# The second head's exponential as two activations, each with its own row sum

## What is computed

```python
B, H, S, D = q.shape          # 4, 8, 1152, 64
q_pool = q.reshape(B, H, S // 2, 2, D).mean(axis=3)
scores = scale * np.matmul(q_pool, k.transpose(0, 1, 3, 2))
scores = scores - np.max(scores, axis=-1, keepdims=True)
attn = np.exp(scores)
attn = attn / (np.sum(attn, axis=-1, keepdims=True) + 1e-09)
out = np.matmul(attn, v)      # then moe(out) and mlp(...)
```

## Time and profile before

| | us |
|---|---|
| median of 3 runs | 886.7 |
| lowest and highest of the 3 | 885.58, 887.46 |
| the profiled execution | 885.63 |
| its span in the trace | 883.8 |
| length of a pair in the middle of attention | 32.9 |

### The profile page before, as it was taken

How to read it: one execution, slowest core, us unless ns; L and a number is a source line. 1 busy time by engine, 2 the same in 40 slices (tenths; PEclk the granted TensorE clock), 3 DMA queues, 4 the chain that set the end, 5 groups by cost and what they waited for, 6 DMA issues and landing times. The chain is left out here.

```text
span 883.8 us, 16411 instructions
## 1 busy us (share of the span) xinstructions
PE 811.5 (92%) x5819; PEld 597.8 (68%) x5819; DVE 531.0 (60%) x984; ACT 483.5 (55%) x729; POOL 248.6 (28%) x154
## 2 busy tenths in 40 slices
PE   3899999999999999999999988878678999999998
PEld 3676776776667677676677665634236888888886
DVE  2666666666666766766766754430037667677663
ACT  2566566566566566566566554220048666766672
POOL 2304304404404403403403300000038344334432
PEclk9999999999999999999999999979889999999999
DMA  5353303303303303303303164348960000000000
GB/s 134 131 145 81 81 2 82 80 1 80 80 0 80 80 0 80 80 0 80 80 0 80 63 252 162 125 170 315 404 253 1 25 24 24 24 24 24 24 24 24
DMA packets 82160, 75.49 MB, mean 85 GB/s; under 512 B 42448, under 2 KB 60880, under 8 KB 81616
## 3 DMA queue, kind: packets, MB, share of 16 engines
q1 hardware_dynamic: 79792, 74.47, 26.5%
q10 hardware_dynamic: 2336, 0.59, 0.3%
HBM read 70.32 MB, written 4.72 MB: 85 GB/s over the span
## 5 line engine op out<-in xcount | busy, mean ns | idle before, releaser
L493 ACT ACTIVATE prob<-ps,neg_max 128x1152 f32<-128x1152 f32 x144 | 175.7, 1221 | 186.6 <-DVE spare L402 186.6
L290 PE MATMUL ps<-ident,prob 128*128 128x128 f32 x1296 | 169.7, 280 | 29.3 <-ACT prob L493 27.1
L290 PEld LDWEIGHTS ps<-ident,prob 128*128 128x128 f32 x1296 | 140.7, 142 | 72.5 <-ACT prob L493 63.9
L306 PE MATMUL ps<-probT,v_nat 128*64 128x256 f32 (+1 forms) x1152 | 153.6, 411 | 0.0
L398 DVE TENSOR_REDUCE part_neg<-ps 128x1 f32<-128x512 f32 x160 | 109.7, 692 | 45.7 <-PE ps L259 38.2
L372 DVE COPY probT<-ps 128x128 f32<-128x128 f32 (+1 forms) x192 | 75.5, 421 | 99.5 <-PE ps L290 99.5
L466 ACT ACTIVATE probT<-ps 128x512 f32<-128x512 f32 x208 | 117.1, 594 | 32.1 <-PE ps L290 32.0
L208 POOL TENSOR_TENSOR kT<-k_raw,ones 128x1152 fp32r<-128x1152 f32 x15 | 31.6, 2107 | 311.0 <-DVE k_raw L448 311.0
L259 PE MATMUL ps<-kT,qT_hi 64*128 64x512 f32 (+1 forms) x768 | 112.2, 369 | 2.6 <-DVE qT_lo L389 2.6
L306 PEld LDWEIGHTS ps<-probT,v_nat 128*64 128x64 f32 x1152 | 77.3, 136 | 52.2 <-issue 5.7
L963 PE MATMUL ps<-w_hi,g_even 128*128 128x512 f32 x320 | 102.6, 392 | 2.2 <-POOL g_even L1047 2.0
(11 more groups left out here) (144 smaller groups left out, 1038.5 us busy)
## 6 DMA issues: line engine op xcount, KB each, us to landing
slot<-in_moe_w SPq DMA_DIRECT2D x16, 2048.0 KB, 12.8
v_nat<-in_v SPq DMA_DIRECT2D x16, 576.0 KB, 5.0
k_nat<-in_k SPq DMA_DIRECT2D x30, 288.0 KB, 4.0
q_nat<-in_q SPq DMA_DIRECT2D x32, 256.0 KB, 4.1
out<-res SPq DMA_DIRECT2D x18, 256.0 KB, 2.0
slot<-in_moe_w_in SPq DMA_DIRECT2D x2, 2048.0 KB, 20.8
slot<-in_moe_w_out SPq DMA_DIRECT2D x8, 512.0 KB, 16.7
q_nat_r<-in_q SPq DMA_DIRECT2D x32, 32.0 KB, 3.5
```

Source lines behind the costliest of these rows:

```text
L290: last = nc.tensor.transpose(dst[:, n * P:(n + 1) * P], prob[h][:, kt * P:(kt + 1) * P], ident[:])
L306: last = nc.tensor.matmul(ps[64 * h:64 * h + D, VBANK, 0:n], v_nat[par][:, h, kt, :], probT[g][:, kt, h, :], start=(kt == 0), stop=(kt == ...
L493: nc.scalar.activation(prob[h][:], row, ACT.Exp, bias=neg_max[:, j:j + 1], scale=-1.0, accum_out=sums).then_inc(exp_done, 1)
```

## The change

In every round with two heads, the second head's exponential becomes two activations: columns 0 to 511 with the sum into `row_sum`, raising a new semaphore `exp_begun`, and columns 512 to 1151 with the sum into a new small tile `rest_sum`, raising `exp_done`. On PE head 1's first four transposes (chunk 0) wait for `exp_begun`, and its fifth (the first of chunk 1) for `exp_done`. Head 0 and the mix round are as they were. The two sums are added in `invert`, where a tensor_scalar becomes a scalar_tensor_tensor. POOL fills the two new tiles at the start with zeros, and the waits on `zeroed` go from 4 to 6. In the changed kernel L290 is L298, L466 is L474, L493 is L502 with the second piece at L505, and L256 and L259 of before are L259 and L262.

```diff
+        rest_sum = [sb(f"rest_sum{i}", [P, QT + 1, 2]) for i in range(2)]
...
             for i in range(2):
                 nc.gpsimd.memset(row_sum[i][:], 1.0).then_inc(zeroed, 1)
+                nc.gpsimd.memset(rest_sum[i][:], 0.0).then_inc(zeroed, 1)
             nc.gpsimd.memset(ones[:], 1.0).then_inc(zeroed, 1)
-            pool.wait_ge(zeroed, 4)
+            pool.wait_ge(zeroed, 6)
...
                 tau = tiles_of(p, r) + h
-                pe.wait_ge(exp_done, tau + 1)
+                if h == 0:
+                    pe.wait_ge(exp_done, tau + 1)
                 for c in (2, 0, 1) if r == MIX else range(NCH):
                     dst = turned(r, h, c)
+                    if h == 1 and c == 0:
+                        pe.wait_ge(exp_begun, doubles_of(p, r) + 1)
+                    elif h == 1 and c == 1:
+                        pe.wait_ge(exp_done, tau + 1)
...
-                nc.vector.tensor_scalar(row_den[:], row_sum[par][:], 1e-9, None, ALU.add).then_inc(den_done, 1)
+                nc.vector.scalar_tensor_tensor(row_den[:], row_sum[par][:], 1e-9, rest_sum[par][:], ALU.add, ALU.add).then_inc(den_done, 1)
...
+                first = BANK if h == 1 else S
                 row = flat[:, 3 * h * BANK:3 * h * BANK + S]
-                nc.scalar.activation(prob[h][:], row, ACT.Exp, bias=neg_max[:, j:j + 1], scale=-1.0, accum_out=sums).then_inc(exp_done, 1)
+                nc.scalar.activation(prob[h][:, 0:first], row[:, 0:first], ACT.Exp, bias=neg_max[:, j:j + 1], scale=-1.0,
+                                     accum_out=sums).then_inc(exp_begun if h == 1 else exp_done, 1)
+                if h == 1:
+                    nc.scalar.activation(prob[h][:, first:S], row[:, first:S], ACT.Exp, bias=neg_max[:, j:j + 1], scale=-1.0,
+                                         accum_out=rest_sum[par][:, ROUND[r], h:h + 1]).then_inc(exp_done, 1)
```

More of the change, by code:

```diff
@@ L100, in attention @@
         scores_full, neg_done, exp_done = sem("scores_full"), sem("neg_done"), sem("exp_done")
+        exp_begun = sem("exp_begun")
         ktr_full, qtr_full, q_evac, q_high, q_low = (
@@ L317, in turn_out @@
                 last.then_inc(otr_full, 1)
-            pe.wait_ge(zeroed, 4)
+            pe.wait_ge(zeroed, 6)
             pe.wait_ge(ident_ready, 1)
@@ L382, in _ @@
         def _(dve):
-            dve.wait_ge(zeroed, 4)
+            dve.wait_ge(zeroed, 6)
             split(dve, 0)
@@ L468, in _ @@
             load_k(act, 0)
-            act.wait_ge(zeroed, 4)
+            act.wait_ge(zeroed, 6)
             nc.scalar.activation(warm[:], ones[:], ACT.Exp)
@@ L1139, in program @@
                ("outT0", 2 * P + QR), ("outT1", 2 * P), ("ones", 8), ("warm", 8), ("part_neg", 8), ("spare0", P), ("neg_max", 16),
-               ("row_sum0", 16), ("row_sum1", 16), ("mix_sum0", 8), ("mix_sum1", 8), ("row_den", 16), ("row_inv", 16)),
+               ("row_sum0", 16), ("row_sum1", 16), ("rest_sum0", 16), ("rest_sum1", 16), ("mix_sum0", 8), ("mix_sum1", 8), ("row_den", 16), ("row_inv", 16)),
     }
```

## The result

The changed kernel takes 875.68 us (median of 4 runs, 874.87 to 877.19) where the kernel before takes 886.14 (4 runs, 884.62 to 887.46) beside it: a ratio of 0.9884, 95% interval 0.9862 to 0.9907. It was run again later: 875.91 us (6 runs), ratio 0.9888, interval 0.9851 to 0.9926. So it is faster by 10 us, 1.2%. The forecast was 879.0 with a range from 876.0 to 883.5: the right direction and, for most of the gain, the right mechanism, but the gain was over a third larger than forecast (10.5 us against 7.7) and the time lies just under the range.

A forecast was written before the change was run, and what follows sets the result against it. PE bounds the kernel, through its work and gaps in attention. 16 pairs at 0.49 us, less 0.18, give 7.7 us; 886.7 - 7.7 = 879.0 us, forecast case 877.9 to 880.8, range 876.0 to 883.5.

The forecast's parts named there:

- The bound and the ceiling: Attention on PE: blocks of 18 loads against 1.94 us unhindered lose 0.67 us a pair, at most 10.7 us over 16 pairs.
- d: ACT, head 1's exponential: the fixed part of an activation's pitch, which the second activation repeats, taken as 0.25 us.
- The blocks: PE's 18 loads in rounds 0, 1, 3, 4: end at old release + 0.25 + 0.53 us or unhindered, whichever is later.
- The tightest place: Round 1, ACT's copy out of bank 0 before the next scores: covered by only 0.02 us, so nothing lost.
- The sum of the blocks: Attention's 16 pairs at 0.49 us each, less 0.18 for the first pair's round 0: 7.7 us faster.
- Does the rest follow: Everything outside the blocks: copies covered, exponentials move along, the part behind attention moves with its end; no further loss.
- a cheaper activation: Rival on ACT: shorter activations overlap more, d near 0.19, gain 9.5 us, 877.2 us, down to 876; chance 0.12.
- a gain given back: Rival: round 1's gain runs into bank 0 and is lost, gain 4.8 us, 881.9 us, up to 883.5; chance 0.13.
- Nothing: Rival: d near 0.43, or the expert weights set the end instead of attention: 886.7 us; chance 0.08.
- slower: Rival: second piece comes later than d = 0.43, at 0.55 each round ends 0.12 us later: 894.4 us; chance 0.07.

The follow-up runs named there:

- e4: Changed kernel with head 1's pieces in the other order, columns 512 to 1151 first, five transposes ahead of the second wait: 875.70 us, ratio to before 0.9865.
- e3: Changed kernel without the early wait: two activations, but PE waits for the second piece before all nine transposes of head 1: 899.84 us, ratio to before 1.0137.
- e8: Changed kernel with a one-column activation behind the second piece, ahead of the copy out of bank 0: 877.25 us (1 run), pair 32.47 us.
- e2: The kernel before, unchanged, run again for a second trace: 886.90 us, ratio to before 0.9994.
- e5: Kernel before with 18 transposes filling PE's idle time in the last pair's mix round: 888.01 us, ratio to before 0.9987.
- e13: Kernel before with 16 more transposes ahead of the last pair's mix round, moving PE's idle time 1.7 us later: 885.38 us, ratio to before 0.9972.
- e7: Changed kernel with a one-column activation between the two pieces, making the second later: 886.25 us (1 run), pair 32.58 us.
- e9: Changed kernel with a first piece of 256 columns, two transposes on it and seven on the second: 886.93 us, ratio to before 0.9995.
- e14: Changed kernel with 16 more transposes ahead of the last pair's mix round: 879.70 us, ratio to before 0.9916.
- e1: The changed kernel, as it is, run again for a second trace: 875.91 us, ratio to before 0.9888.
- e10: Changed kernel with a first piece of 384 columns, three transposes on it and six on the second: 878.31 us (1 run), pair 32.67 us.
- e12: e4 with 18 idle-time transposes in the last mix round, mix scores' chunk 1 first and the mix exponential split: 885.69 us, ratio to before 0.9980.
- e15: e4 with 18 transposes filling PE's idle time in the last mix round: 876.96 us, ratio to before 0.9900.

## Why the prediction was right or wrong

- **The bound and the ceiling** (PE; the sum of four blocks against 18 unhindered loads): right. e4 reached the ceiling, 1.95 us in every round.
- **d, what the second activation costs ACT**, 0.25 us: 0.24 in the trace, and 0.24 a round as a loss in e3. The estimate from the Trainium skill's figures ("ScalarE: Activation LUTs", section "What ACT_TABLE_LOAD costs"), about 0.19, and its budget of about 0.3 for each ACTIVATE (section "Rules for kernel authors") lie on either side; the trace agrees with neither exactly.
- **The blocks**, forecast 2.01, 2.05, 1.94 and 1.94 us: 1.99, 2.05, 1.95 and 1.95. The rule behind them held at two, three, four and five transposes ahead of the second wait.
- **The tightest place**, bank 0 in round 1 with 0.02 us of cover: right; e8 and e4 ran into it at once.
- **The sum of the blocks**, 7.7 us: mis-sized; the pairs gave 8.75. It was 16 times one pair, the seventh, with 0.49 us; that pair gave 0.52, and eleven of the sixteen gave 0.48 to 0.53. The other five gave more. In the second, fifteenth and last pairs the kernel before lost more in its blocks than in the seventh (2.24, 2.31 and 2.08 us in rounds 0, 1 and 3 of the second, where the seventh has 2.19, 2.23 and 2.05), and they gave 0.57, 0.58 and 0.62. The fourth gave 0.70, since its round 1 came late in the kernel before. Head 0's exponential there:

```profile
125.44 1.22 ACT L493 ACTIVATE prob<-ps,neg_max 128x1152 f32<-128x1152 f32 x1 [2.69 <-DVE spare L402]
```

It starts 7.06 us behind that pair's first exponential (118.38), where the seventh pair needs 6.78; in the changed kernel both need 6.6. The other three traces with a single exponential for head 1 (e2, e5, e13) have the same 7.06; the cause is not known. And the first pair gave 0.63 where 0.31 was forecast: its round 0, which the prediction had dropped since it ran at the lower clock without waiting for head 1, gained too, its 18 loads going from 3.54 us to 3.32, because the lower clock ended at another place.

- **"Does the rest follow"**: this is the step that failed. It took everything outside the blocks as unchanged and PE as at full clock in attention, and so put the clock's part at nothing. The page's slices hold 22 us each and their digit is 9 from 90% up, so a drop of 3.4 us at half clock hardly shows in them. The term that was missing is 1.40 us in the last mix round; with the blocks' 1.05 and 0.36 us from the start and behind attention it makes the difference between 7.7 and 10.5. The range's lower end was the ceiling of the blocks, which a term outside the blocks can pass. A further 0.6 us of the miss in time is the base: the forecast started from 886.7, the median of three runs, and the kernel before had 886.14 over the four beside the changed one.
- **The rivals**: a cheaper activation and a gain given back were wrong by d and by the pair's length. The first of them has the times nearest to the measured one (877.2, down to 876), but by luck: its mechanism did not act. "Nothing" and "slower" hung on d of 0.43 and more, where 0.24 was measured; e7 shows that a second piece 0.10 us later costs 0.20 us a pair, as the rule for the blocks has it. The other ground for "nothing", that the expert weights set the end, is ruled out by the stretch behind attention, 342.35 us before and 342.02 after.

What stays open: what the place of an idle time has to be measured against for the lower clock to follow it, and how often in the timed runs either kernel has the drop in the last mix round. In the traces without filling it was there in eight (before, e2, e3, e4, e7, e8, e9, e14) and not in four (the changed kernel, e1, e10, e13). Open as well is when the clock falls behind attention. In eleven traces that stretch takes 341.7 to 342.5 us and is at full clock for its first 34 us; in six (e2, e5, e7, e8, e12, e15) the clock also falls 11 to 12 us behind the last exponential, for 3.4 to 13.7 us, and the stretch takes 342.9 to 349.7.

## What to carry to other kernels

Splitting a producer pays by what no longer waits for its last piece, not by how early the consumer starts: work out the end as old release, plus the fixed cost of one more instruction, plus the work still behind the last wait, and look for the split (or the order of the pieces) that leaves least behind it. Before sizing such a gain, measure several periods of the loop and not one. And when a change shortens the path to an idle stretch of TensorE, the clock behind it may go either way: compare the granted clock at that place in both traces before crediting the change. Removing one drop does not settle it either: look whether another has come up further on.

## What the runs showed of the hardware

- An idle time of 2.6 us on TensorE, between stretches of dense work, was followed by 3.4 us at 1.2 GHz in some traces and by none in others, in the first pair even with the same code (the idle time that ends at 28.04 us in the trace of before has none behind it, the one that ends at 28.88 in e2 has one). In the last mix round moving it by 1.7 us switched the drop on in one kernel and off in the other, and filling it with transposes removed it. A drop of 3.4 us cost 1.3 to 1.4 us there (7.16 to 7.26 against 5.83), and the 6.8 us of e7 cost 2.6 (8.44).
- ACT starts the next activation about 0.10 us into the accumulator read of 0.19 to 0.20 us, also when that next one accumulates too. An activation with pointer bias and accumulator, from its start to the next one's, takes about 0.24 us plus 0.84 ns a column (0.68, 0.77 and 1.21 us for 512, 640 and 1152 columns); one of a single column, with neither, takes 0.10 us (e7, e8).
- PE's 18 loads take the same time with a third wait among them as with two, if it is already met when they get there: 1.95 us in round 4 of the changed kernel against 1.96 before.
